# A third value product in three passes, and one more operand on GpSimd, in a fused attention and MLP kernel

## The reference

```python
q_rot, k_rot = (rotate(q), rotate(k))
scores = scale * np.matmul(q_rot, k_rot.transpose(0, 1, 3, 2))
scores = scores - np.max(scores, axis=-1, keepdims=True)
attn = np.exp(scores)
attn = attn / (np.sum(attn, axis=-1, keepdims=True) + 1e-09)
out = np.matmul(attn, v)
# x: (2304, 512), heads side by side
h = x @ w_in                               # 512 -> 1024
solu = h * softmax(h)
ln = (solu - mean) / np.sqrt(var + 1e-06) * g_ln
return ln @ w_out                          # 1024 -> 512
```

## Time and profile before

| What | Value |
|---|---|
| Median of three runs | 483.8 us |
| Profiled execution | 483.53 us |
| Its span, first to last instruction | 481.8 us |
| TensorE busy | 473.4 us, 98% of the span |
| VectorE, ScalarE, GpSimd busy | 79%, 52%, 49% |
| TensorE on the chain that ended last | 95% of the span |
| Mean granted TensorE clock | 1.000 |

### The profile page before, as it was taken

One profiled execution on the slowest core, in us unless ns is written; L12 is line 12 of the kernel. 1 busy time (PEld: TensorE's weight loads), 2 busy tenths in 40 slices (PEclk: granted clock), 3 DMA queues, 4 the chain that ended last, 5 costly groups with the idle time before them and its releaser, 6 DMA issues.

```text
span 481.8 us, 7983 instructions
## 1 busy us (share of the span) xinstructions
PE 473.4 (98%) x2553; PEld 402.9 (84%) x2553; DVE 381.4 (79%) x591; ACT 250.4 (52%) x397; POOL 236.1 (49%) x307
## 2 busy tenths in 40 slices
PE   7899999999999999999999999999999999999997
PEld 7678888988898889888888878888888888888885
DVE  6867898889889888988896366999897899888731
ACT  4667677777777777777777352032223222322221
POOL 6877666867686768667772021342352121222110
PEclk9999999999999999999999999999999999999999
DMA  8503544645455545445424203233333233322242
GB/s 295 188 12 77 151 147 113 184 131 168 101 156 164 161 116 152 145 123 169 135 71 100 68 6 59 34 83 69 85 87 62 51 51 68 80 57 60 59 81 84
DMA packets 101009, 50.61 MB, mean 105 GB/s; under 512 B 90280, under 2 KB 90280, under 8 KB 99048
## 3 DMA queue, kind: packets, MB, share of 16 engines
q1 hardware_dynamic: 100152, 50.00, 38.7%
q10 hardware_dynamic: 816, 0.10, 0.1%
HBM read 33.33 MB, written 4.79 MB: 79 GB/s over the span
## 4 chain that ended last, share of the span: by engine, by line
PE 95%; DVE 2%; ACT 1%; DMA 1%; issue 0%; SPq 0%; DVEq 0%; ACTq 0%
PE ps L1169 20%; PE ps L1183 20%; PE ps L1155 20%; PE ps L1106 18%; PE ps L1077 8%; PE ps L1135 4%; PE ps L1121 4%; DMA X<-x_in 1%; DVE nm L843 1%; DVE X L780 1%; DVE QK L816 0%; DVE X L785 0%; ACT QK L595 0%; ACT p_main L650 0%; ACT QK L610 0%
## 5 line engine op out<-in xcount | busy, mean ns | idle before, releaser
L843 DVE TENSOR_REDUCE nm<-ps 128x1 fp32r<-128x576 f32 x144 | 108.1, 755 | 31.7 <-PE ps L1077 29.1
L1155 PE MATMUL ps<-p_main,V 128*128 128x288 f32 x404 | 114.8, 406 | 0.0
L1169 PE MATMUL ps<-w_hi,KB 128*128 128x512 f32 x288 | 91.5, 390 | 0.0
L1183 PE MATMUL ps<-w_hi,QK 128*128 128x512 f32 x288 | 91.0, 389 | 0.0
L1106 PE MATMUL ps<-QK 128*128 128x288 f32 x320 | 90.0, 362 | 0.8 <-ACT p_main L650 0.5
L650 ACT ACTIVATE p_main<-ps 128x576 f32<-128x576 f32 x101 | 65.7, 651 | 42.6 <-PE ps L1106 41.2
L1155 PEld LDWEIGHTS ps<-p_main,V 128*128 128x128 f32 x404 | 71.0, 190 | 10.8 <-ACT p_main L650 0.2
L412 POOL TENSOR_TENSOR X<-X,rope 128x1152 f32<-128x1152 f32 x26 | 68.5, 2660 | 10.8 <-POOL v_lo_b L453 8.2
L1106 PEld LDWEIGHTS ps<-QK 128*128 128x128 f32 x320 | 55.6, 189 | 17.9 <-issue 5.7
L1106 PE MATMUL ps<-KB 128*128 128x288 f32 x320 | 67.8, 293 | 0.0
L486 POOL COPY V<-oe 32x256 f32<-32x256 f32 x72 | 29.8, 413 | 74.2 <-DVE QK L894 41.6
(11 more groups left out here) (118 smaller groups left out, 717.8 us busy)
## 6 DMA issues: line engine op xcount, KB each, us to landing
X<-x_in SPq DMA_DIRECT2D x13, 1152.0 KB, 5.1
V<-oe SPq DMA_DIRECT2D x213, 32.0 KB, 1.9
V<-v_in SPq DMA_DIRECT2D x32, 160.0 KB, 2.8
out<-X SPq DMA_DIRECT2D x18, 256.0 KB, 2.3
w_raw<-w_in SPq DMA_DIRECT2D x16, 256.0 KB, 2.9
xT<-x_in SPq DMA_DIRECT2D x2, 1152.0 KB, 10.2
xT<-oe SPq DMA_DIRECT2D x16, 144.0 KB, 2.4
inv<-inv_rows SPq DMA_DIRECT2D x16, 144.0 KB, 3.0
```

What stands on the lines that cost most here:

```text
L843: nc.vector.tensor_reduce(nm[g][:, at:at + 1], src[:, :, 0:HALF], AX_XY, ALU.max, negate=True)\
L1155: ins = nc.tensor.matmul(o_ps[a][:, half, 0:HALF], v, p[:, half * HALF:(half + 1) * HALF], start=(k == 0), stop=(k == 9))
L1169: ins = nc.tensor.matmul(h_ps[t % 3][:, half, :], left[a][:, c, :], right[:, col:col + 512], start=(c == 0 and k == 0), stop=(c == KC - 1 ...
L1183: ins = nc.tensor.matmul(y_ps[a], left[a][:, c * P:(c + 1) * P], right[:, col:col + 512], start=(i == 0), stop=(i == DOWNS - 1))
```

## The change

A third product, k = 1, joins `HALVED`, in pairs 2 to 14. Each halved product gets its own pair of tiles `v_hi`, `v_lo` (before: one pair for each head). ScalarE empties output tile b before exp of step 1, since that exp is now written there. The low queries of head b of pair n+1 move, for n of 2 to 14, from VectorE's step 1 to GpSimd, ahead of the rotation; `low_p` of product 1 takes their place on VectorE. GpSimd splits v for products 1 and 3 right after the rotation, for product 8 where it did before. In the opening the low queries of head a of pair 0 move to GpSimd, ahead of the low keys of head b; VectorE makes the low keys ahead of the second queries; and the row scores of the first four tiles of pair 0 use the high parts alone, 64 rows, without a wait for low keys and second queries.

```diff
-HALVED = (3, 8)
+HALVED = (1, 3, 8)
@@ GpSimd, opening
+            pool.wait_ge(hi_done[0], 1)
+            pool.wait_ge(low_k_done[0], 1)
+            low_queries(0, 0)
             pool.wait_ge(first_hi_k[1], 1)
             pool.wait_ge(low_q_done[0], 1)
             low_keys(0, 1)
...
@@ GpSimd, iterations
-            halve_v(1, 0)
+            halve_v(1, HALVED[1])
             for n in range(1, PAIRS):
+                if n == 1:
+                    pool.wait_ge(low_q_done[1], 3)
+                elif n + 1 < PAIRS:
+                    pool.wait_ge(low_k_done[1], n + 2)
+                    pool.wait_ge(hi_done[1], high(n + 1, 1))
+                    pool.wait_ge(low_q_done[1], n + 1)
+                    low_queries(n + 1, 1)
+                    pool.wait_ge(low_q_done[1], n + 2)
                 if n + 2 < PAIRS:
-                    pool.wait_ge(low_q_done[1], n + 2)
...
                     rotate(n + 2)
+                for k in HALVED[0:2]:
+                    if halved(n + 1, k):
+                        halve_v(n + 1, k)
                 if n + 2 < PAIRS:
                     pool.wait_ge(rot_done, n + 3)
                     high_keys(n + 2, 0)
...
-                if halved(n + 1, HALVED[0]):
-                    halve_v(n + 1, 0)
-                    halve_v(n + 1, 1)
+                if halved(n + 1, HALVED[2]):
+                    halve_v(n + 1, HALVED[2])
@@ ScalarE
+                    if s == HALVED[1] and n >= 2:
+                        act.wait_ge(pv_done, PVS * n + HALVED[0] + 1)
...
+                    if s == 1 and n >= 2:
+                        take_o(n - 1, 1)
                     exp(n, s)
...
-                        if s == 1:
-                            take_o(n - 1, 1)
+                        if s == 1 and n == 1:
+                            take_o(0, 1)
@@ VectorE, opening and steps
             first_add(0, rot_done)
+            low_keys(0, 0)
             first_second_queries()
-            low_keys(0, 0)
-            low_queries(0, 0)
...
-                    if s == 1:
-                        low_queries(n + 1, 1)
+                    if s == 1 and halved(n, HALVED[0]):
+                        low_p(n, HALVED[0])
+                    if n == 1 and s == 1:
+                        low_queries(2, 1)
@@ TensorE, row_scores
-                if i == 0:
+                if i == 0 and m == 0:
+                    pe.wait_ge(hi_done[0], 1)
+                    pe.wait_ge(first_hi_k[0], 1)
+                elif i == 0:
...
+                elif m == 0 and i < BOTH:
+                    parts = [(QK[0][own(0), 0, i * P:(i + 1) * P], QK[0][own(0), 1, 0:S])]
```

More of the change, by code:

```diff
@@ L89, in attention_then_mlp @@
         p_lo = sb("p_lo", [P, S], F32R)
-        v_hi = [sb(f"v_hi_{h}", [P, P], F32R) for h in "ab"]
-        v_lo = [sb(f"v_lo_{h}", [P, P], F32R) for h in "ab"]
+        v_hi = [sb(f"v_hi{i}", [P, P], F32R) for i in range(len(HALVED))]
+        v_lo = [sb(f"v_lo{i}", [P, P], F32R) for i in range(len(HALVED))]
         oe = [sb(f"oe{c}", [P, 2, S]) for c in range(2)]
@@ L104, in attention_then_mlp @@
         p_lo_done = sem("p_lo_done")
-        v_hi_done = [sem(f"v_hi_{h}_done") for h in "ab"]
-        v_lo_done = [sem(f"v_lo_{h}_done") for h in "ab"]
+        v_hi_done = [sem(f"v_hi{i}_done") for i in range(len(HALVED))]
+        v_lo_done = [sem(f"v_lo{i}_done") for i in range(len(HALVED))]
         second_done = sem("second_done")
@@ L218, in halved, with halves, head @@
         def halved(n, k):
-            return k in HALVED and (1 if k == HALVED[0] else 2) <= n < PAIRS - 1
-        def halves(n, a):
-            return 2 * (n - 1) + a + (1 if n == 1 else 0)
+            return k in HALVED and (1 if k == HALVED[1] else 2) <= n < PAIRS - 1
+        def halves(n, k):
+            i = HALVED.index(k)
+            return 1 if n == 1 else 3 * (n - 2) + i + 2
+        def head(k):
+            return k // 5
         def high(m, a):
@@ L442, in set_tails, with halve_v @@
                 pool.wait_ge(tails_set, 3 * m)
-            def halve_v(m, a):
+            def halve_v(m, k):
+                i, a = HALVED.index(k), head(k)
+                first = 1 if i == 1 else 2
                 pool.wait_ge(v_loaded[m % 2], uses(m) * 32)
[L447 to L455, removed]
+                if m > first:
+                    pool.wait_ge(pv_done, PVS * (m - 1) + k + 1)
+                    pool.wait_ge(v_lo_done[i], m - first)
+                v = V[m % 2][:, a, (k - 5 if a else k + 1), own(a)]
+                nc.gpsimd.tensor_copy(v_hi[i][:, own(a)], v).then_inc(v_hi_done[i], 1)
+                pool.wait_ge(v_hi_done[i], m - first + 1)
+                nc.gpsimd.tensor_tensor(v_lo[i][:, own(a)], v, v_hi[i][:, own(a)].bitcast(F32), ALU.subtract)\
+                  .then_inc(v_lo_done[i], 1)
+                pool.wait_ge(v_lo_done[i], m - first + 1)
             def high_keys(m, a):
@@ L503, in _ @@
                 nc.gpsimd.memset(V[c][:, 1, :, 0:D], 1.0).then_inc(v_const, 1)
[L504 to L507, removed]
+            for i, k in enumerate(HALVED):
+                nc.gpsimd.memset(v_hi[i][:, other(head(k))].bitcast(F32), 1.0).then_inc(v_const, 1)
+                nc.gpsimd.memset(v_lo[i][:, other(head(k))].bitcast(F32), 0.0).then_inc(v_const, 1)
+            pool.wait_ge(v_const, 10)
             nc.gpsimd.memset(expo[:, :], -0.5).then_inc(const_done, 1)
@@ L789, in first_second_queries @@
                 dve.wait_ge(rot_done, 1)
+                dve.wait_ge(hi_done[0], 1)
                 nc.vector.tensor_copy(QK[0][other(0), 0, 0:S], x_of(0)[own(0), 1, :]).then_inc(hi_done[0], 1)
@@ L851, in row_max, with low_p @@
                     nc.vector.transpose(nm_row[g][:, :], nm[g][:, :].bitcast(F32)).then_inc(turned[g], 1)
-            def low_p(n, a):
-                dve.wait_ge(p_hi_done, halves(n, a))
+            def low_p(n, k):
+                a = head(k)
+                dve.wait_ge(p_hi_done, halves(n, k))
                 nc.vector.tensor_tensor(p_lo[:, :].rearrange("p (b c) -> p b c", b=2), o_ps[1 - a][:, :, 0:HALF],
@@ L970, in _ @@
                         low_keys(n + 1, 1)
-                    if s == 1:
-                        low_queries(n + 1, 1)
+                    if s == 1 and halved(n, HALVED[0]):
+                        low_p(n, HALVED[0])
+                    if n == 1 and s == 1:
+                        low_queries(2, 1)
                     if s == 4 and n >= 2:
                         w_low(n - 1)
-                    if s == 3 and halved(n, HALVED[0]):
-                        low_p(n, 0)
+                    if s == 3 and halved(n, HALVED[1]):
+                        low_p(n, HALVED[1])
                     if n == 1 and s == 7:
                         w_low(0)
-                    if s == 7 and halved(n, HALVED[1]):
-                        low_p(n, 1)
+                    if s == 7 and halved(n, HALVED[2]):
+                        low_p(n, HALVED[2])
                     if s == 5 and n + 2 < PAIRS:
@@ L1055, in row_scores @@
                     pe.wait_ge(low_k_done[0], m + 1)
+                    pe.wait_ge(pool_const, 7)
+                if i == BOTH and m == 0:
+                    pe.wait_ge(hi_done[0], 2)
+                    pe.wait_ge(low_k_done[0], 1)
                     pe.wait_ge(pool_const, 7)
@@ L1125, in weigh_tails, with weigh_halves @@
                             ins.then_inc(pv_done, 1)
[L1127 to L1133, removed]
+            def weigh_halves(n, k):
+                i, a = HALVED.index(k), head(k)
+                pe.wait_ge(v_lo_done[i], n if i == 1 else n - 1)
+                pe.wait_ge(p_hi_done, halves(n, k))
+                for part, (v, p) in enumerate(((v_hi[i], p_hi), (v_lo[i], p_hi), (v_hi[i], p_lo))):
+                    if part == 2:
+                        pe.wait_ge(p_lo_done, halves(n, k))
                     for half in range(2):
@@ L1141, in weigh @@
                     if half == 1:
-                        weigh_halves(n, k // 5)
+                        weigh_halves(n, k)
                     return
@@ L1148, in weigh @@
                         pe.wait_ge(v_loaded[c], uses(n) * 32)
-                        pe.wait_ge(v_const, 8)
+                        pe.wait_ge(v_const, 10)
                         pe.wait_ge(max_taken, STEPS)
```

## The result

The changed kernel takes 488.48 us (median of five runs, 487.25 to 490.44) against 483.8 us: a ratio of 1.0099, interval 1.0075 to 1.0123. Slower, as forecast, but by 4.7 us where 2.6 were expected, and above the range's end of 488.2. The profiled execution took 489.39 us, with a span of 487.6 us and a mean granted TensorE clock of 0.992. The five runs go with their clocks: 487.25 us at 1.000, 487.86 and 488.48 at 0.996, 489.39 at 0.992, 490.44 at 0.989. At full clock the loss is thus 3.5 us (one run), inside the range; the clock brings it to between 4.1 and 6.6 us in the other four.

The account below looks back on a forecast made before the run. TensorE bounded the pairs at 16.48 us; the loop of GpSimd and VectorE, 16.75, was to become the bound. Pairs +2.0 and opening +0.6 gave +2.6 on 483.53, 486.1, plus 0.27 for the median: 486.4 us, range 481.7 to 488.2.

Parts of the forecast that it names:

- the loop of GpSimd and VectorE: In the pairs: waits on the shared port lock make it 16.75 us, above the 16.29 TensorE wants, so it bounds.
- the opening: Pair 0: tile 4 waits for GpSimd's low keys, score (0, 0) moves from 16.15 to 16.7: +0.6 us.
- the pairs: Pairs' rotation falls back 0.27 us an iteration, +2.6; less 0.43 of slack and 0.19 from pair 14: +2.0 us.
- The saving of 0.19 us: Product 1 in three passes instead of float32, pairs 2 to 14: 0.19 us less TensorE time each, 2.4 us.
- the lateness of ScalarE: `take_o` ahead of exp of step 1 delays the next scores by 0, bound 0.05 a pair, 0.7 us.
- H: Start of the first `high_keys` in GpSimd's loop, forecast at R + 2.85; from there to the next R 13.90 us.
- R: End of the rotation in GpSimd's loop, the point from which the forecast counts the loop.
- The loop that fits: Rival in the pairs: GpSimd and VectorE need 16.29 us or less, so faster, 482.0 us; chance 0.22.
- The even loop: Rival in the pairs: both splits ready before the addition, loop 16.45 us, gain lost, 483.7 us; chance 0.13.
- The other order: Rival in the pairs: addition starts ahead of the second split in all, 16.96 us, 488.7; other orders' chance 0.17.
- the lock ahead of the low keys: Rival: `second_queries` beats VectorE's low keys to the lock, loop grows 0.1, 487.5 us; other orders' chance 0.17.
- The opening that gains: Rival in pair 0: tile 4 isn't what decides, 0.5 us less instead of 0.6 more; no chance of its own.

Follow-up runs that it names:

- the opening alone: The kernel before with only the opening's part of the diff: 485.81 us, ratio 1.0044.
- the gap filled: Kernel before with only the new opening, plus eight extra 128x128 matmuls of no use ahead of tile 4: 485.09 us, ratio 1.0019.
- keys first: Kernel before with only the new opening, GpSimd making low keys of head b ahead of low queries of head a: 484.31 us, ratio 1.0012.
- the pairs alone: The change without its opening, against the kernel before: 487.05 us, ratio 1.0064.
- ScalarE's part: The change without its opening, with ScalarE instead of GpSimd making the high parts of v for products 1, 3 and 8: 483.32 us, ratio 0.9987.

## Why the prediction was wrong

**What held.** Slower was right, and for the reason given: the loop of GpSimd and VectorE became the bound of the pairs. Two terms of the sum were too small, the opening and the pairs. At full clock the miss is 0.9 us (487.25 against 486.4, one run), and most of that is the pairs; the rest, up to 3.2 us more, is the clock.

**The opening, the largest error in the profiled execution.** Forecast +0.6, measured +3.1 in the profiled execution (2.8 without the later load). The mechanism and its part at full clock held: tile 4 waits for GpSimd's low keys, GpSimd's low queries were held by VectorE's copy (1.58 instead of 1.41 us, from 11.32 to 12.90; that the copy is the cause is read from their times, not tested), tile 4's maximum 0.6 late. The term that was mis-sized is the last one: I gave the wait its length and no more. It left TensorE idle for 1.2 us, and the granted clock then was 0.50 for about 3.4 us in the opening alone (up to 18.0) and some 7 here (up to 22.7), where TensorE's scores are on the path. The opening alone lost 0.45 us in the run whose clock stayed, and 1.5 to 4 us in the others; with the gap filled the spread was gone. Whether the 64-row matmuls or the wait ahead of the first row scores help to bring the clock down stays open (keys first). My bounds for the opening (-0.5 to +0.75) had no clock in them.

**Product 1.** The saving of 0.19 us was mis-sized. The pass with low p comes 0.14 late, as `low_p` ends at 110.13 for matmuls that would have run from 110.30 with their weights loaded 0.26 sooner: the product takes 0.94, not 0.80.

```profile
109.37 0.76 DVE L881 TENSOR_TENSOR p_lo<-ps,p_hi 128x576 fp32r<-128x576 f32 x1 [0.23 <-ACT p_hi L668]
```

I had put the lateness of ScalarE at 0 with a bound of 0.05, and checked it only against the next scores, not against `low_p` behind it. TensorE's own pair is 16.44 us.

**The loop of GpSimd and VectorE.** Right in mechanism, place and size: 16.75 forecast, 16.78 measured, with H at R + 2.80 (2.85) and 13.98 from H to R (13.90). `w_low` waits for the rotation, the last subtraction for the addition, `second_queries` for the low keys, each as worked out. That this loop makes the loss of the pairs, and not the new products, is shown by the pairs alone, where it stays without the new opening, and by ScalarE's part: with the same products, and the high parts made elsewhere, the loss is gone. Part of that gain came from less work on GpSimd and part from the waits around it; the two were not told apart.

**The sum for the pairs.** Forecast +2.0, measured +2.8. The rotation of iteration 3 was 0.15 late where I had it 0.08 early (0.2); the ten after it lost 0.30 each and not 0.27 (0.3); and pair 14 gave next to nothing of its 0.19, since its product saves 0.04 (0.15). The rest, 0.1, is in the slack I gave TensorE and in rounding. Without the new opening it is +3.0: there the addition went ahead of the second split once, at 0.3. That the orders could change from pair to pair I had only as two separate cases.

**The rivals.** The loop that fits, at 482.0, needed 16.29 us and fell. The even loop fell (16.8). The other order came in no pair of this kernel and once in the pairs alone; that its 488.7 lies near the 488.48 measured is chance. `second_queries` never got the lock ahead of the low keys in the rows shown (119.37 against 119.34). The opening that gains fell: the early maxima were lost at tile 4, and in the kernel with keys first at the rotation.

## What to carry to other kernels

Sum an engine's loop in order, with every exclusive hold by its neighbour, not by its idle time: GpSimd had 4 us idle a pair and 2.2 us of work to take, and the loop still came out 0.3 us over the old pace. Where a change makes the matrix engine wait 1 us or more on the path, price the clock as well as the wait, look at the spread of the runs against their clocks, and fill the gap if nothing else can (here that took the spread away, and was still 1.0 us slower than the kernel before). Before a product is made cheaper, follow its operands' last producer: here the copy of high parts, the subtraction behind it and the exp of the step left 0.04 of 0.19 us.

## What the runs showed of the hardware

An idle stretch of 1.2 us on TensorE brought 3.4 us at half clock in the trace of the opening alone and some 7 in that of the kernel after, with another wait, of 1.5 and 0.7 us, some 3 us ahead of it. The clock fell 0.2 us before the stretch ended in the one, and 1.1 us behind it in the other. In four runs of five of either kernel the mean clock was under 1.000, in the fifth it was not: the same kernel ran with means of 1.000 and of 0.989, 3 us apart. That agrees with the Trainium skill, TensorE: Matmul & The Clock Gate, section "What's actually happening", by which activity sets the clock of the array and the default state is the slow one. One wait of 1.27 us in the opening of the kernel before brought nothing of the kind (0.999 or 1.000 in all 45 runs beside the experiments). Why a gap of this length was enough in some executions and not in others no run here shows. And the second split started 0.02 to 0.04 us ahead of the addition in 22 pairs of the kernel after and the pairs alone together: it won in 21 of them, and lost in one, at 0.3 us.
